# Transposes of a unit's activations at other places in TensorE's order

## What is computed

```python
def _moe2_ref(x, w_skip, w_gate, w1, w2):        # x 2304 x 512, 8 experts, 512 -> 1024 -> 512
    do_compute = x @ w_skip > 0
    out = x.copy()
    xc = x[do_compute]
    logits = xc @ w_gate
    e_idx = np.argmax(logits, axis=1)
    ...                                           # gate_w: softmax weight of the chosen expert
    for e in range(E):
        mask = e_idx == e
        h = np.maximum(xc[mask] @ w1[e], 0.0)
        y[mask] = gate_w[mask, None] * (h @ w2[e])
    out[do_compute] = xc + y
```

## Time and profile before

| | |
|---|---|
| time, median of 3 runs | 750.23 us (750.04 to 750.71) |
| the profiled execution: time | 749.35 us |
| its span, first to last instruction | 747.6 us |
| mean granted clock of TensorE | 0.992 of full speed |
| PE busy in the span | 726.1 us, 97% |
| units of experts 1 to 7 | 18, from 655.2 us to 741 us of the span |

### The profile page before, as it was taken

One profiled execution on the slowest core, in us unless ns is written; L12 is line 12 of the kernel. 1 busy time (PEld: TensorE's weight loads), 2 busy tenths in 40 slices (PEclk: granted clock), 3 DMA queues, 4 the chain that ended last, 5 costly groups with the idle time before them and its releaser, 6 DMA issues.

```text
span 747.6 us, 16594 instructions
## 1 busy us (share of the span) xinstructions
PE 726.1 (97%) x6083; PEld 581.6 (78%) x6083; DVE 344.4 (46%) x831; ACT 286.7 (38%) x736; POOL 163.1 (22%) x200
## 2 busy tenths in 40 slices
PE   7999999999999999999999999999999999979996
PEld 4555878778787887898888787888787869868885
DVE  6776554464445543012345465555556273212221
ACT  5566664465354643233423222222222131223332
POOL 3226554333113321100020000000000013234443
PEclk9999999999999999999999999999999999989998
DMA  4335766644555532376657767777765217694850
GB/s 129 100 121 166 224 197 192 190 133 138 147 150 146 145 97 73 103 204 176 190 174 218 203 199 184 204 184 211 188 213 126 76 44 262 257 340 164 295 198 10
DMA packets 116772, 126.55 MB, mean 169 GB/s; under 512 B 23854, under 2 KB 79934, under 8 KB 116712
## 3 DMA queue, kind: packets, MB, share of 16 engines
q1 hardware_dynamic: 113768, 121.37, 55.4%
q0 software_dynamic: 2048, 3.80, 1.6%
q10 hardware_dynamic: 896, 0.59, 0.3%
HBM read 88.66 MB, written 35.52 MB: 166 GB/s over the span
## 4 chain that ended last, share of the span: by engine, by line
PE 91%; DVE 3%; issue 2%; DMA 2%; ACT 1%; DVEq 0%; POOL 0%; POOLq 0%; SPq 0%; ACTq 0%
PE ps_h L1889 9%; PE ps_x L1976 9%; PE ps_x L1978 9%; PE ps_x L1977 9%; PE ps_h L1891 9%; PE ps_h L1890 9%; PE ps_o L1872 6%; PE ps_t L1846 5%; PE ps_y L2203 5%; PE ps_hid L2186 4%; PE ps_hid L2153 3%; PE ps_s L1797 2%; PE ps_s L1833 2%; PE ps_s L1834 2%; PE ps_s L1790 1%
## 5 line engine op out<-in xcount | busy, mean ns | idle before, releaser
L1889 PE MATMUL ps_h<-xh,win_h 128*128 128x512 f32 (+1 forms) x320 | 122.9, 384 | 1.0 <-ACT act L1187 0.8
L1891 PE MATMUL ps_h<-xh,win_l 128*128 128x512 f32 (+1 forms) x320 | 118.3, 370 | 0.0
L1890 PE MATMUL ps_h<-xl,win_h 128*128 128x512 f32 (+1 forms) x320 | 118.0, 369 | 0.0
L1976 PE MATMUL ps_x<-wout_h,g_hi 128*128 128x512 f32 x288 | 114.1, 396 | 0.0
L1978 PE MATMUL ps_x<-wout_h,g_lo 128*128 128x512 f32 x288 | 112.4, 390 | 0.0
L1977 PE MATMUL ps_x<-wout_l,g_hi 128*128 128x512 f32 x288 | 112.2, 389 | 0.0
L1173 ACT ACTIVATE prob<-ps_s,neg_max 128x128 f32<-128x128 f32 (+3 forms) x144 | 79.1, 551 | 55.9 <-DVE neg_max L1401 38.6
L1401 DVE TENSOR_REDUCE neg_max<-ps_s 128x1 f32<-128x128 f32 (+3 forms) x144 | 71.0, 509 | 59.4 <-PE ps_s L1834 35.7
L1187 ACT ACTIVATE act<-ps_h 128x512 f32<-128x512 f32 (+1 forms) x80 | 44.4, 556 | 123.6 <-PE ps_h L1891 116.7
L1441 DVE TENSOR_TENSOR g_lo<-g_raw,g_hi 128x512 fp32r<-128x512 f32 x72 | 49.4, 687 | 48.1 <-ACT g_hi L1197 48.0
L1889 PEld LDWEIGHTS ps_h<-xh,win_h 128*128 128x128 f32 x320 | 60.4, 189 | 11.5 <-issue 1.4
(11 more groups left out here) (230 smaller groups left out, 1024.1 us busy)
## 6 DMA issues: line engine op xcount, KB each, us to landing
arena<-in_w SPq DMA_DIRECT2D x64, 512.0 KB, 6.8
g_raw<-hidden SPq DMA_DIRECT2D x72, 256.0 KB, 4.2
hidden<-act SPq DMA_DIRECT2D x64, 256.0 KB, 2.4
k_raw<-in_k_t SPq DMA_DIRECT2D x40, 144.0 KB, 3.1
x2rows<-x_both SPq DMA_DIRECT2D x18, 256.0 KB, 2.3
out<-x_both SPq DMA_DIRECT2D x18, 256.0 KB, 2.6
x2quarters<-x_both SPq DMA_DIRECT2D x18, 256.0 KB, 4.2
w_stage<-in_w_in SPq DMA_DIRECT2D x16, 256.0 KB, 2.9
```

Of the source, the lines that this page charges most:

```text
L1889: e.matmul(dst, win_h[:, f, kc, :], xh[m][:, kc, :], start=kc == 0, stop=False)
L1890: e.matmul(dst, win_h[:, f, kc, :], xl[m][:, kc, :], start=False, stop=False)
L1891: last = e.matmul(dst, win_l[:, f, kc, :], xh[m][:, kc, :], start=False, stop=kc == KC - 1)
L1976: e.matmul(dst, hi, wout_h[:, f, :], start=f == 0, stop=False)
```

## The change

The transpose of half 0 stands ahead of the last k of half 1 of the first product, so that 28 of the product's 32 matmuls come before it and 4 behind it. The transpose of half 1 stands inside half 0 of the second product, behind its k = 1: 8 of 32 matmuls come before it. Each keeps its wait on `q_relu`. The transpose of the next unit's rows stays between the two products. No instruction is added or removed, and nothing changes on the other engines.

```diff
                     for half in range(2):
                         for k in range(KC):
+                            if half == 1 and k == KC - 1:
+                                e.wait_ge(q_relu, 2 * u + 1)
+                                e.transpose(ps_ht[0][:, 0:P], hid_q[:, 0, :], ident[:, :]).then_inc(q_ht, 1)
                             for c, own in enumerate(lanes):
...
                         last.then_inc(q_hid, 1)
-                    e.wait_ge(q_relu, 2 * u + 1)
-                    e.transpose(ps_ht[0][:, 0:P], hid_q[:, 0, :], ident[:, :]).then_inc(q_ht, 1)
                     transpose_unit(u + 1)
-                    e.wait_ge(q_relu, 2 * u + 2)
-                    e.transpose(ps_ht[1][:, 0:P], hid_q[:, 1, :], ident[:, :]).then_inc(q_ht, 1)
                     e.wait_ge(q_first, u + 1)
                     e.wait_ge(q_out, u + 1)
...
                         for k in range(4):
+                            if half == 0 and k == 2:
+                                e.wait_ge(q_relu, 2 * u + 2)
+                                e.transpose(ps_ht[1][:, 0:P], hid_q[:, 1, :], ident[:, :]).then_inc(q_ht, 1)
                             for c, own in enumerate(lanes):
```

## The result

The changed kernel takes 755.44 us (median of 4 runs, 754.41 to 756.22) against 750.47 us before (4 runs too, one more than in the table of before; 750.04 to 751.04): ratio 1.0064, 95% interval 1.0049 to 1.0079, so 3.7 to 5.9 us slower. Forecast were 755.6 us in a range of 752.7 to 757.5, slower. The profiled execution took 756.22 us, its span is 754.4 us.

The account below looks back on a forecast made before the run. TensorE's own order was taken to bound the unit loop. Changes of array form 4.25, less long waits 0.60, plus unit 1 0.9 and a new wait 0.85, gave +5.4 us: 755.6 us on the timed scale, range 752.7 to 757.5.

Parts of the forecast that it names:

- What bounds the loop: Unit loop: bound by TensorE's own order, 4.36 us from one first product to the next in an ordinary unit.
- A trip costs time by itself: Each extra change from 32-column tiles to a full-array transpose and back costs TensorE 0.19 us; +0.25 a unit in all.
- The wait for the copy of half 1: Second product: a new wait for the copy to `hid_tq` behind half 1's moved transpose, 0 to 0.11 us, taken as 0.05 a unit.
- The ReLU's waits go: Half 1's transpose no longer awaits its ReLU: 0.13 us saved in each unit, about 0.15 more in four.
- No wait on the other two hand-overs: Half 0's transpose doesn't await its ReLU (0.2 us to spare); VectorE's copy of half 0 is hidden by 0.13.
- Unit 1, +0.9: Unit whose half 0 transpose waits 3.67 us for ScalarE, then runs mostly at 1.2 GHz: +0.77 to +0.97 us, taken as 0.9.
- Unit 2: Counted among the 17 units at full clock, each +0.25 us without the new wait.
- A: Transposes apart among tiles cost nothing extra, a lone one 0.17 us: net -2.4, 747.8 us; 6 in 100.
- B: Only entering the full array costs, 0.10 us; the way back is hidden, a lone transpose takes 0.27: +2.8, 753.0 us; 12 in 100.
- C: Unit 1's long wait or its clock moves: 752.9 us (6 in 100) if the clock keeps up, 757.4 (5) if the wait grows.
- D: Moved transposes lose and gain nothing, slack meeting the costs: within 1.5 us of 750.2; 6 in 100.

Follow-up runs that it names:

- half 0 alone: Kernel before with only half 0's transpose moved, ahead of the last k of the first product; 755.82 us in one run (before 749.09).
- rows alone: Kernel before with only the next rows' transpose moved, behind k = 1 of half 0 of the second product; 756.96 us in one run (before 749.09).
- half 1 alone: Kernel before with only half 1's transpose moved, into the second product behind its k = 1; 755.15 us in one run (before 749.09).
- two trips, little wait: Kernel before, half 0's transpose ahead of the first product's last two k, the other two together behind the second's k = 1; 750.24 us (before 749.56).
- one k sooner: Changed kernel with half 1's transpose behind k = 0 of the second product, not k = 1; 790.61 us on a chip where the kernel before took 790.36.
- one k later: Changed kernel with half 1's transpose behind k = 2 of the second product, not k = 1; 780.62 us on a chip where the kernel before took 790.36.
- the tiled kernel at the old places: Kernel before, each transpose made of four matmuls on 32-column tiles, places unchanged; 789.63 against 790.36 us, on another chip 749.63 against 749.56.

## Why the prediction was right, step by step

With the pace of 0.109 us a wave and 0.17 us for a transpose in a row of them, the units of all kernels with full-array transposes add up in one way: 32 waves 3.49, three transposes 0.51, together 4.00, and then a price for each trip and the waits.

| kernel | trips | wait in a unit | unit | price of a trip: (unit - 4.00 - wait) / trips |
|---|---|---|---|---|
| before | 1 | 0.13, ReLU of half 1 | 4.36 | 0.23 |
| changed | 3 | none | 4.69 | 0.23 |
| half 0 alone | 2 | 0.30, ReLU of half 1 | 4.76 | 0.23 |
| rows alone | 2 | 0.30, ReLU of half 1 | 4.76 | 0.23 |
| half 1 alone | 2 | 0.34, copy of half 0 | 4.74 | 0.20 |
| two trips, little wait | 2 | 0.06, small ones | 4.46 | 0.20 |

The waits are differences of starts: 0.30, 0.47 and 0.47 us where 0.17 would do, and in the fifth line 697.02 - 696.48 = 0.54 where 0.20 would do (the row's 0.27 counts from the modelled end of the transpose). The 0.20 is what the tiles take after the second of two transposes in a row with no wait between them (699.99 to 700.19). The last two kernels each have one such pair, and a trip with it costs 0.17; the other trip costs 0.23, and the column has their mean. So a trip has two prices, by whether its last transpose's weights were loaded ahead.

- **What bounds the loop: right.** The move of a transpose to which nobody pays heed changed every unit by 0.40 us.
- **A trip costs time by itself: right, its size low.** 0.19 was taken from before (0.10 in, 0.09 back); 0.23 it is. Starts read to the nanosecond in the changed kernel give the missing 0.04: the first wave after the return takes 0.134 us where the others take 0.109, and from the last wave to the transpose it is 0.223, so 0.11 over the pace and not 0.10. Two waves and an entry take 703.00 - 702.64 = 0.36 us, where 0.22 + 0.10 were reckoned. In the kernel before, the longer first wave of the second product was hidden in the pace of 0.11 that I drew from 1.77 / 16; the pace is 0.109.
- **The wait for the copy of half 1, 0.05 us a unit: wrong.** It is nothing in the changed kernel (one k sooner brings nothing, one k later costs 0.20). 17 x 0.05 = 0.85 us were booked there; the under-sized trips, two more a unit, are 17 x 0.08 = 1.4 us. The two errors go against each other.
- **The ReLU's waits go: right.** 0.13 in every unit. Of the longer ones the row of waits gave four; the distances of the first products give the same four of 14, with 0.13 to 0.14 more, and none after. Over these 14 units: 0.25 + 0.05 a unit less 0.56 (four of them) would be +3.6; measured +4.0, which is 0.33 a unit.
- **No wait on the other two hand-overs: right.** L2186 waits in unit 1 alone, and the second product for VectorE's copy in no ordinary unit.
- **Unit 1, +0.9: near, with its parts off.** From its first transpose (667.53) to the next first product (672.64) it takes 5.11 us, 4.32 before: +0.79, in the bounds of 0.77 to 0.97. But the way from a lone transpose to the tiles, reckoned at 0.35, takes 0.40 at the low clock (667.53 to 667.93, where 0.35 before was that of the last of three in a row). At the low clock throughout it would have been +1.05; the full clock came back at 672.4, ahead of the last waves, which took 0.26 back. The gather came 0.27 later against the start of the unit, inside of the 0.3 added for it. These are the rows of after:

```profile
667.53 0.48 PE L2186 MATMUL ps_ht<-ident,hid_q 128*128 128x128 f32 x1 [4.15 <-ACT hid_q L1315]
667.93 0.65 PE L2189 MATMUL ps_hid<-arena,rows_tq 128*32 128x128 f32 x8
...
672.64 1.70 PE L2189 MATMUL ps_hid<-arena,rows_tq 128*32 128x128 f32 x56
```

- **Unit 2, missed.** I gave it +0.25, and it came out 0.61 us shorter. Before, its first product still began at the low clock (2.78 us from its start to the transpose, 1.86 at full pace); after, it runs at full pace from its start (1.64 us to the transpose). That is 0.92 us. Unit 1 lasts longer and takes more of the low clock into itself; and the low clock began earlier against unit 1's work. These are the stretches at half clock, before and after (columns as in the earlier trace rows); in the 1 us on either side the granted clock was 0.98 to 1.00:

```profile
664.60:671.40 6.80, 6.18 (x103) 5.34 (x107) 1.39 (x6) 1.80 (x8) 1.36 (x2) 0.50 1.03 406
665.50:672.40 6.90, 4.87 (x67) 3.26 (x71) 0.89 (x4) 1.71 (x7) 1.04 (x1) 0.51 1.03 410
```

  They are equally long, but 0.6 us of the first and 2.0 us of the second lay ahead of unit 1's first transpose, where TensorE waited for the gather anyway. So 1.4 us less of it fell on work, worth 0.7 us. Why it fell earlier stays open, and these are one execution each.
- **The rivals.** A (a lone transpose costs 0.17) fell to the pauses and to the rows' transpose moved alone. B (only the way in costs) fell to the same kernel: 0.40 and not 0.27. C (the long wait or its clock moves) came true in part: the 0.7 us of the bullet above, of its 2.7. D fell with the measurement.

The sum by what was measured in the two executions: +0.31 + 1.06 - 0.61 + 4.01 + 0.30 = 5.07 us, for 5.4 forecast; the medians differ by 4.97. That the two are so near is partly luck: 1.4 us were missing for the size of the trips, 0.85 were booked for a wait that isn't there, and units 1 and 2 together came to +0.45 where +1.15 was booked. 5.4 + 1.4 - 0.85 - 0.7 is 5.2. The direction and most of the size rest on the trips, and those the experiments show.

## What to carry to other kernels

Ahead of moving a full-array transpose, or any full-array matmul, into a stretch of tiled ones to fill a wait, count the changes of the array's form and price each from a place in the same trace that has one: here a wait of 0.13 us was bought off with two more trips at 0.23. Keep the full-array pieces together even if one of them waits, and look for the wait inside such a group, where other full-array work fills it for nothing, before looking among the tiles. Giving up the full-array form is no clear gain either: with no trips at all the unit came only from 4.36 to 4.33 us. The trip's 0.23 is gone, but six tiled waves take 0.65 us for 0.50 of three transposes, and the waits for the ReLU of half 1 and the copy of half 0 grow by 0.05.

## What the runs showed of the hardware that was not expected

- The tiles' first wave after a full-array instruction takes 0.134 us to the next and not 0.109. It needs no full-array instruction: in the tiled kernel at the old places the two waves that start after the wait for the ReLU (698.26 to 698.50) take 0.24 us, the two at 697.68 take 0.22. In both cases the weight loads start together with the wave and not ahead of it.
- After two transposes in a row the tiles follow 0.20 us behind the second (699.99 to 700.19) and not 0.26: the second's weights were loaded ahead, at 699.90, under the first. The Trainium skill, page "TensorEngine Tiling (Array Packing)", section "Key Properties", has the drain without a price; here in and out together are 0.23 us at 2.4 GHz, 0.17 with such a pair.
- Full-array f32 transposes 128x128 among full-array matmuls follow each other at 0.11 us (612.99 to 613.43 for four). The 0.17 us in a row of the unit loop is what the second takes behind one that has just come out of the tiles.
- Four f32 matmuls on 32-column tiles against the identity transpose 128x128 in 0.22 us of start to start, against 0.17 for the full-array form in a row and 0.40 for one alone among tiles. Alone among tiles, the tiled form is the cheaper one.
- The kernel before took 749.1 to 750.5 us in three sets of runs and 790.4 us on one other chip. The tiled kernel at the old places was profiled both there and elsewhere: its unit loop begins at 654.8 and 656.8 us and takes 132 and 90 us, so the difference lies in the unit loop, where ScalarE and VectorE stand still on that chip by what the profile calls "remote". What it is stays open.
